# Two more levels of a gated linear attention with one 128-row product per chunk for two heads

## The reference

```python
state = 0
for t in range(S):                       # B, H, S, D = 4, 8, 768, 48
    cur = einsum('bhd,bhe->bhde', u * k[t], v[t])
    y[t] = einsum('bhd,bhde->bhe', r[t], state + cur)
    state = w[t][..., None] * state + einsum('bhd,bhe->bhde', k[t], v[t])
x = y as (B*S, H*D) = (3072, 384)
```

## Time and profile before

| what | us |
|---|---|
| median of 3 runs | 555.84 |
| lowest and highest of them | 555.8, 557.96 |
| the profiled execution's own time | 555.19 |
| its span, first to last instruction | 553.4 |
| PE, DVE, ACT busy in it | 485.5, 334.6, 332.8 |

### The profile page before, as it was taken

The page is one execution under the profiler, slowest core; times in us unless marked ns, Lnnn a source line. Parts: engine busy times, 40 slices in busy tenths (PEclk is TensorE's granted clock), DMA queues, the critical chain, the costliest instruction groups (busy, mean ns, idle before and its releaser), DMA issues.

```text
span 553.4 us, 18757 instructions
## 1 busy us (share of the span) xinstructions
PE 485.5 (88%) x7850; PEld 425.1 (77%) x7850; DVE 334.6 (60%) x583; ACT 332.8 (60%) x689; POOL 13.7 (2%) x21
## 2 busy tenths in 40 slices
PE   1778889798989898678698879999999999999996
PEld 0557768677777777667333469999999999999996
DVE  5688868587878788925341167555555555555552
ACT  1787677686868687434221276656565656565653
POOL 9000000000000000000000000000000000000000
PEclk9998989798989899959889979999999999999999
DMA  6885565736262621293799730101010101010101
GB/s 112 146 213 103 150 113 152 137 70 117 57 118 52 114 56 34 59 403 136 238 390 369 260 114 1 44 1 44 1 43 2 43 0 43 0 43 1 44 1 43
DMA packets 119788, 56.23 MB, mean 102 GB/s; under 512 B 102944, under 2 KB 116256, under 8 KB 119328
## 3 DMA queue, kind: packets, MB, share of 16 engines
q1 hardware_dynamic: 116512, 42.54, 31.1%
q10 hardware_dynamic: 3200, 12.58, 6.1%
HBM read 50.38 MB, written 4.72 MB: 100 GB/s over the span
## 4 chain that ended last, share of the span: by engine, by line
PE 72%; ACT 11%; issue 7%; SPq 4%; DVE 4%; DMA 0%; ACTq 0%; DVEq 0%
PE bank L707 12%; PE bank L708 12%; PE bank L709 12%; ACT wide L802 4%; PE ybank L485 4%; PE lbank L468 4%; PE ybank L501 4%; PE lbank L451 4%; PE bank L697 4%; SPq L289 4%; PE tbank L402 3%; PE tbank L415 2%; PE bank L646 2%; PE bank L623 2%; ACT wl L743 2%
## 5 line engine op out<-in xcount | busy, mean ns | idle before, releaser
L707 PE MATMUL bank<-wo_high,h_high 128*128 128x384 f32 x384 | 129.6, 337 | 1.8 <-DVE h_low L1207 1.6
L708 PE MATMUL bank<-wo_low,h_high 128*128 128x384 f32 x384 | 129.0, 336 | 0.0
L709 PE MATMUL bank<-wo_high,h_low 128*128 128x384 f32 x384 | 128.9, 336 | 0.0
L953 ACT ACTIVATE h_relu<-bank 128x384 f32<-128x384 f32 x128 | 62.9, 492 | 74.4 <-PE bank L697 74.1
L1205 DVE CAST h_high<-h_sq 128x384 fp32r<-128x384 f32 x128 | 46.0, 359 | 96.7 <-PE bank L709 88.0
L1041 DVE TENSOR_TENSOR rk<-rk,wl 112x768 f32<-112x768 f32 x80 | 76.3, 954 | 36.7 <-PE lbank L468 19.9
L707 PEld LDWEIGHTS bank<-wo_high,h_high 128*128 128x128 f32 x384 | 72.6, 189 | 3.2 <-issue 2.7
L1207 DVE TENSOR_TENSOR h_low<-h_sq,h_high 128x384 fp32r<-128x384 f32 x128 | 71.5, 558 | 4.5
L708 PEld LDWEIGHTS bank<-wo_low,h_high 128*128 128x128 f32 x384 | 72.7, 189 | 0.0
L709 PEld LDWEIGHTS bank<-wo_high,h_low 128*128 128x128 f32 x384 | 72.5, 189 | 0.0
L957 ACT ACTIVATE h_sq<-h_relu 128x384 f32<-128x384 f32 x128 | 67.4, 527 | 4.1
(11 more groups left out here) (123 smaller groups left out, 532.5 us busy)
## 6 DMA issues: line engine op xcount, KB each, us to landing
w_sb<-in_moe_w_dram ACTq DMA_DIRECT2D x8, 1536.0 KB, 8.7
w_hi<-in_moe_w_dram SPq DMA_DIRECT2D x16, 384.0 KB, 8.0
nat<-in_w_dram SPq DMA_DIRECT2D x64, 72.0 KB, 2.4
nat<-in_r_dram SPq DMA_DIRECT2D x64, 72.0 KB, 2.5
nat<-in_k_dram SPq DMA_DIRECT2D x64, 72.0 KB, 2.4
v_tok<-in_v_dram SPq DMA_DIRECT2D x32, 144.0 KB, 3.1
w_lo<-in_moe_w_dram SPq DMA_DIRECT2D x1, 4608.0 KB, 16.8
out_dram<-o_sb SPq DMA_DIRECT2D x8, 576.0 KB, 3.0
```

Source lines behind the costliest of these rows:

```text
L707: nc.tensor.matmul(acc, hi, wo_high[:, fb, :], start=(fb == 0), stop=False)
L708: nc.tensor.matmul(acc, hi, wo_low[:, fb, :], start=False, stop=False)
L709: last = nc.tensor.matmul(acc, lo, wo_high[:, fb, :], start=False, stop=(fb == NF - 1))
L953: nc.scalar.activation(h_relu[fb % 2][:], h_bank[fb % 2][:, 0:GT * P], ACT.Relu).then_inc(relu_done, 1)
```

## The change

Levels 4 and 5 are added to `WIDE`. So they make 12 products of 128 rows in place of 24 of 64; for level 5 the weights are cut to 32 columns. Five levels instead of three are spread, so ACT's order gets four more calls of `widen`, each two copies. The result of level 5 now stands at the start of `lbank[s]`. The zeros of `wide[s]` are as before: each head's copies go to the same place.

```diff
-    WIDE = (1, 2, 3)
+    WIDE = (1, 2, 3, 4, 5)
@@ level
                     pe.wait_ge(widened[s], 2 * (len(WIDE) * rd + WIDE.index(lv) + 1))
+                    rows = C if lv < 5 else SUB
                     for c in range(NC):
                         i, par = divmod(c, 2)
-                        dst = lbank[s][C * par:C * par + C, 0:2 * PER * SUB].rearrange("p (h x) -> p h x", h=2)
-                        last = nc.tensor.matmul(dst[:, :, SUB * i:SUB * i + SUB], src[:, 1, C * c:C * c + C],
+                        dst = lbank[s][C * par:C * par + rows, 0:2 * PER * SUB].rearrange("p (h x) -> p h x", h=2)
+                        last = nc.tensor.matmul(dst[:, :, SUB * i:SUB * i + SUB], src[:, 1, C * c:C * c + rows],
                                                 wide[s][:, :, SUB * c:SUB * c + SUB], start=True, stop=True)
@@ top_level_out
-                    src = lbank[s][rows, 512 - PER * SUB:512 + PER * SUB].rearrange("p (n t) -> p n t", t=SUB)
+                    at = 0 if 5 in WIDE else 512 - PER * SUB
+                    src = lbank[s][rows, at:at + NB * SUB].rearrange("p (n t) -> p n t", t=SUB)
@@ the order on ACT, in a round
                 widen(rd, 1, 3)
                 if ahead:
                     inputs_out(rd + 1, 6, 1)
+                widen(rd, 0, 4)
                 if late:
                     y_to_x(rd - 1, 0)
                 if ahead:
                     inputs_out(rd + 1, 7, 1)
+                widen(rd, 1, 4)
                 for s in range(2):
                     spread_w(rd, s)
...
                 if ahead:
                     inputs_out(rd + 1, 8, 2)
+                widen(rd, 0, 5)
                 if ahead:
                     inputs_out(rd + 1, 10, 1)
+                widen(rd, 1, 5)
                 top_level_out(rd, 0)
```

## The result

The changed kernel takes 561.88 us in the median of 20 runs, against 555.65 us for the kernel before, measured beside it: ratio 1.0111, 95% interval 1.0091 to 1.0130. It is slower by 1.1%, 6.2 us. The forecast was slower, 559.3 us, in a range of 550 to 568.

What follows compares the result with a forecast made beforehand. The prediction took ACT, which hands over each attention round, as the bound; round changes, with round 7 at -1.5, summed to +3.45 us, giving 558.6 profiled and a 559.3 us median. The range was 550 to 568 us.

Steps and rivals of the forecast that it cites:

- ACT as the one that hands over: Attention rounds: ACT's top-level copy of s = 1 comes about 1.3 us late, making a round 29.3 us.
- The first pair of copies: ACT, level 4 of s = 0: the pair ends at 119.9, before PE's wait ends at 120.26, so costs nothing.
- The sum over rounds 0 to 6: Attention rounds 0 to 6: per-round changes of +1.0, +0.3, -0.4, +0.8, +1.1, +0.75 and +1.4 us.
- PE's cost of the products: PE, levels 4 and 5: wide products add 0.02 and 0.22 us per level, 0.5 us per round, off the path.
- the array rule: PE, levels 4 and 5: narrow products up to 2x faster, so wide ones cost 0.43 us more each; rival, 563 us, chance 0.04.
- 0 on the path: PE, levels 4 and 5: the products' extra 0.5 us per round lies ahead of and beside ACT's handover.
- Rival B: Attention rounds: instruction supply was the bound, all stalls go and copies fit into room; rounds 28.1 us, 548 us, chance 0.14.
- The stalls: PE's issue waits: gone or absorbed in rounds 3 to 6, about 0.5 us left in round 2 under the w1 load.
- mostly hidden: PE's instruction fetch: the skill's claim for crossing a 16 KiB block; the forecast disagreed, citing stalls of 3.21 us.
- Round 7: Last attention round: 2.7 us gained without stalls, 0.4 if a late delivery takes back 2.3; middle taken, 1.5 us gained.
- Rival A, the clock: PE in attention: clock falls at new idle places, 1.2 us a round, +8.4 over 7 rounds, 568 us; chance 0.13.

Runs made afterwards that it cites:

- copies_only: The changed kernel with its copies and PE's wait for them, but narrow 64-row products at levels 4 and 5: 562.16 us, ratio 1.0128 to the kernel before.
- the GpSimd version: The changed kernel with the spreading copies of levels 4 and 5 on GpSimd instead of ACT: 550.93 us, ratio 0.9924 to the kernel before.

## Why the prediction was right, and where it was not

**ACT as the one that hands over: right, and in round 3 to the tenth.** Predicted: level 0 (s 1) 17.6 us into the round, then 11.7, rounds of 29.3. Measured in round 3: 17.68 and 11.66, 29.34. Rounds 4 and 5 have 17.73 and 17.70, and then about 12.1 and 11.9. The first pair of copies (level 4, s 0) was indeed free: it ran from 118.73 in a gap that had been 1.45 us and is now 0.36. `copies_only` shows the mechanism, the GpSimd version its reverse, with the clock in it.

**The sum over rounds 0 to 6: right.** Round 0 +0.9 (forecast +1.0), round 1 -0.2 (+0.3), round 2 -0.8 (-0.4), round 3 +0.9 (+0.8), round 4 +1.6 (+1.1), round 5 +1.1 (+0.75), round 6 +1.8 (+1.4): 5.3 us against 4.95. Some of this is luck: rounds 1 and 2 ran at PEclk 1.00, where they had 0.94 and 0.89 before, and no term of the forecast held that. In the changed kernel with all five loads late, rounds 3 and 4, the same work, took 28.34 us at 1.00 and 29.82 at 0.94. By that difference, an estimate, rounds 1 and 2 would have been longer than forecast at the old clock.

**PE's cost of the products, and the array rule.** Level 5 wide took 0.79 to 0.82 on the chain, where 0.85 was taken. The rule of the Trainium skill, TensorEngine Tiling (Array Packing), "Theoretical Speedup", by which the narrow products would be up to twice as fast, has no support here: 48 narrow records of level 4 took 0.83 us and 24 wide ones 0.85, and the wide products alone are 1% faster. "0 on the path" was right for the change as made, but the same step hid that the products by themselves are a gain of 5 us or so. Rival B had that size, at 548, and it needs the copies to be free; but B had rounds of 28.1 us, where those measured are 26.7 at PEclk 1.00 and 28.15 at 0.94.

**The stalls: right in rounds 3 to 6,** where they went. With the narrow products and the copies, stalls of 1.78 and 1.72 us are back in rounds 4 and 5, at the same matmuls as before, and with the w1 loads away those of round 7 fell to 0.58 and 0.84. So they go by the number of instructions and by the traffic beside them, as late blocks of instructions would; no run shows the blocks themselves arrive. If that is what they are, "mostly hidden" (the Trainium skill, Runtime: NRT & Kernel Launch, "Instruction fetch mechanics") does not hold here.

**Round 7: the step that failed.** The forecast said "4.81 - 2 x 1.07 = 2.7 us gained if no stall is left", and took -1.5 for the round. Level 5 of s = 1 did come 2.7 us earlier in the round (12.4 us after level 3 of s = 0, against 15.1). But up to `k_times_v` nothing was gained: 22.0 us against 21.5. The v load, issued at y_far (s 0) and 15.5 us under way beside w1, sets that point, and the stalls of before had only hidden it. I had read the stalls and not asked what would be late next. That the load was issued 1.3 us later in the round, after a stretch at the low clock, is part of this one execution: with GpSimd's copies there was no such stretch, and `k_times_v` came 20.1 us after level 3, still set by the v load (227.9 + 15.1 = 243.0, and 243.00). So some 1.4 of the 2.7 us were to be had beside the w1 loads, an estimate from that one run. Round 7 is 2.1 us of the missing 3; another 0.5 came behind it, most of it at the second `k_times_v` (1.20 us against 0.74), which ran at the low clock after the stall. Sum: 5.3 + 0.6 + 0.5 = 6.4, as the spans have it.

**Rival A, the clock,** was no further cause in rounds 3 to 5, with a PEclk of 0.94 in each before and after. It did show in round 7, as above. Level 5 alone ran at 0.89 in rounds 3 to 5; that this is the rest of its cost fits the rows and is not shown.

## What to carry to other kernels

A copy added to an engine of 74% occupancy is neither free nor paid in full: what counts is where the engine waits in its own order ahead of the point that hands over the work, and only the waits behind the copy's place can take it up. When an instruction or a load is made faster, look for the transfer that is next at the same point: here the v load took back all that the vanished stalls gave, and with the w1 loads moved the DMA issues on ACT and then w2 took back half. When two kernels are compared by their rounds, compare rounds at the same granted clock too. An idle engine for the helper copy turned a loss of 1.1% into a gain of 0.8%, and with the loads moved 1.6%.

## What the runs showed of the hardware

A 144 KB load in short rows took 2.5 to 3.7 us to land with the w1 loads away and 13.2 to 15.5 us beside w1 loads of 1.5 MB each, which moved some 400 GB/s. The issue of five w1 loads kept ACT from its copies for 3.0 us. GpSimd's copy of 48 x 384 fp32 elements took 530 ns in the row above, as fast as ACT's. One that started beside a TENSOR_TENSOR of DVE took 1.12 us, and its pair 1.68; `w_pairs`, beside such a copy, went from 2.67 to 2.90 us.
